# Two Gram products of the later chunk pairs moved behind an inverse product, and their copies split over ScalarE and VectorE

## The reference

```
# 1. delta-rule attention, k normalised, state S per batch and head
for t in range(S):
    y[t] = q[t] @ state
    state += beta[t] * outer(k_n[t], v[t] - k_n[t] @ state)
# 2. feed forward with three input matrices
x2 = max(x @ w1, x @ w2, x @ w3) @ w_out
# 3. mixture of 8 experts, top 2 by noisy gate
out[token] += weight * (relu(x2[token] @ we1[e]) @ we2[e])
```

## Time and profile before

| | us |
|---|---|
| median of 3 runs (1025.57 to 1025.75) | 1025.73 |
| the profiled execution's own time | 1025.56 |
| its span, first to last instruction | 1023.8 |
| attention ahead of the loop, about | 0 to 67 |
| loop over the tiles, about | 67 to 521 |
| experts | 521 to 1024 |

### The profile page before, as it was taken

One profiled execution on the slowest core, in us unless ns is written; L12 is line 12 of the kernel. 1 busy time (PEld: TensorE's weight loads), 2 busy tenths in 40 slices (PEclk: granted clock), 3 DMA queues, 4 the chain that ended last, 5 costly groups with the idle time before them and its releaser, 6 DMA issues.

```text
span 1023.8 us, 25726 instructions
## 1 busy us (share of the span) xinstructions
PE 997.9 (97%) x10425; PEld 929.1 (91%) x10425; DVE 721.6 (70%) x1701; ACT 469.7 (46%) x700; POOL 214.8 (21%) x229
## 2 busy tenths in 40 slices
PE   8899999999999999999999999999999999999995
PEld 7888898898888888888899999999999999999995
DVE  7988795893884786543569677778677686776772
ACT  4542345226325325233363546546465465654651
POOL 0464310210120130121315221212211112212111
PEclk8899999999999999999999999999999999999998
DMA  9540320420430330116656625234352526526221
GB/s 306 129 109 2 94 53 23 129 61 3 126 85 3 78 93 2 57 42 217 220 188 179 186 43 169 47 88 122 53 156 47 170 39 172 163 55 169 40 30 24
DMA packets 71190, 101.68 MB, mean 99 GB/s; under 512 B 28608, under 2 KB 59584, under 8 KB 70720
## 3 DMA queue, kind: packets, MB, share of 16 engines
q1 hardware_dynamic: 59024, 78.10, 25.4%
q0 software_dynamic: 10992, 20.70, 10.5%
q10 hardware_dynamic: 1088, 1.65, 0.5%
HBM read 136.98 MB, written 29.51 MB: 163 GB/s over the span
## 4 chain that ended last, share of the span: by engine, by line
PE 92%; DVE 3%; ACT 3%; issue 2%; POOLq 0%; POOL 0%; ACTq 0%; DVEq 0%
PE ps L1895 43%; PE ps L2061 20%; PE ps L1944 8%; PE ps L1744 3%; PE ps L2072 3%; PE ps L1874 2%; PE ps L1850 2%; PE ps L1725 2%; PE ps L1862 2%; PE ps L1960 2%; PE ps L1784 1%; DVE prod L1176 1%; DVE x L1180 1%; PE ps L1830 1%; ACT solve L862 1%
## 5 line engine op out<-in xcount | busy, mean ns | idle before, releaser
L1895 PE MATMUL ps<-xr,wr_in 128*128 128x512 f32 x972 | 235.8, 396 | 0.3 <-ACT xr L888 0.3
L1895 PEld LDWEIGHTS ps<-xr,wr_in 128*128 128x128 f32 x972 | 178.6, 188 | 39.6 <-DVE wr_in L1298 0.5
L1895 PE MATMUL ps<-xbT,w1r 128*128 128x256 f32 x1728 | 211.6, 283 | 0.6
L1895 PEld LDWEIGHTS ps<-xbT,w1r 128*128 128x128 f32 x1728 | 209.7, 192 | 2.5 <-issue 2.1
L2061 PE MATMUL ps<-w2r,hbT 128*128 128x384 f32 x1152 | 205.9, 336 | 0.0
L2061 PEld LDWEIGHTS ps<-w2r,hbT 128*128 128x128 f32 x1152 | 198.9, 188 | 0.0
L754 POOL DMA_INDIRECT out_rows<-yb,idx x55 | 91.5, 1664 | 374.8 <-DVE yb L1524 289.1
L965 ACT ACTIVATE hbT<-ps 128x512 fp32r<-128x512 f32 x96 | 57.3, 597 | 166.6 <-PE ps L1895 163.4
L1336 DVE TENSOR_TENSOR w1r<-w1s,w1r 128x768 fp32r<-128x768 f32 x124 | 117.3, 956 | 17.2 <-ACT w1r L949 15.1
L949 ACT CAST w1r<-w1s 128x768 fp32r<-128x768 f32 x124 | 101.2, 828 | 24.8 <-DMA w1s<-in_we 24.8
L1336 DVE TENSOR_TENSOR w2r<-w2s,w2r 128x768 fp32r<-128x768 f32 x124 | 110.2, 950 | 2.0 <-ACT w2r L953 2.0
(11 more groups left out here) (232 smaller groups left out, 1125.6 us busy)
## 6 DMA issues: line engine op xcount, KB each, us to landing
w1s<-in_we SPq DMA_DIRECT2D x31, 1536.0 KB
w2s<-in_we SPq DMA_DIRECT2D x31, 1536.0 KB
xb<-rows SPq DMA_DIRECT2D x24, 402.0 KB
kv_s<-in_kv SPq DMA_DIRECT2D x24, 384.0 KB, 3.7
k_s<-in_k SPq DMA_DIRECT2D x12, 512.0 KB, 4.0
joint<-in_q SPq DMA_DIRECT2D x24, 256.0 KB
out_rows<-padrow SPq DMA_DIRECT2D x13, 384.0 KB, 4.3
w_in<-in_w_blocks SPq DMA_DIRECT2D x3, 1152.0 KB, 9.7
```

What stands on the lines that cost most here:

```text
L1895: mm = pe.matmul(dst, w, m, start=(opens and n == 0), stop=(closes and n == len(todo) - 1))
```

## The change

In every pass that has them, both Gram products of the next pair stand directly behind an inverse product: behind `low_times_inverse(1)` in pass 0 (place 10), behind `corner(cp)` in passes 1 to 3 (place 2). From chunk 4 on even chunks write banks 6 and 7 (`D_BANKS`), odd ones banks 2 and 3 (`C_BANKS`), and the two waits of `gram` go. VectorE copies the blocks of the even chunk, in later passes at place 3, and ScalarE those of the odd one at the corner's place. In pass 0 who copies what, and where it stands, remains. The numbers of semaphore waits inside the copies follow, and `scaled_v` and the start of the early elimination steps are written by other names at the same places.

```diff
         def gram_banks(c):
-            return {1: H_BANKS, 2: H_BANKS, 3: D_BANKS, 4: D_BANKS, 5: C_BANKS}.get(c, E_BANKS)
+            if c < 4:
+                return (E_BANKS, H_BANKS, H_BANKS, D_BANKS)[c]
+            return C_BANKS if c % 2 else D_BANKS
...
-            spread = {"low": 1, "corner": 2, "gram0": 3, "gram1": 4, "k0": 5, "u0": 7, "s0": 8, "k1": 10, "u1": 12,
+            spread = {"low": 1, "corner": 2, "gram": 2, "k0": 5, "u0": 7, "s0": 8, "k1": 10, "u1": 12,
                       "s1": 13}
-            tight = {"low": 1, "corner": 2, "gram0": -1, "gram1": 0, "k0": 4, "u0": 5, "s0": 6, "k1": 7, "u1": 8,
+            tight = {"low": 1, "corner": 2, "gram": 1, "k0": 4, "u0": 5, "s0": 6, "k1": 7, "u1": 8,
                      "s1": 9}
...
-            low, first = place(n - 1, "low"), place(n - 2, "gram1") + 4
+            low, first = place(n - 1, "low"), place(n - 2, "corner") + 6
...
# ScalarE
-                act.wait_ge(s_blk, c + 1 if c < 4 else c)
+                act.wait_ge(s_blk, c + 1 if c < 4 else c // 2 + 3)
...
                         if i == place(t, "corner"):
                             corner(cp)
-                            if t == 0:
-                                diagonals_of(5)
-                        if t and i == place(t, "gram0") and cp + 1 < CP:
-                            diagonals_of(c + 2)
-                        if t and i == place(t, "gram1") and cp + 1 < CP:
-                            diagonals_of(c + 3)
+                            if cp + 1 < CP:
+                                diagonals_of(c + 3)
...
# VectorE
-                dve.wait_ge(s_half_diag, 3)
+                dve.wait_ge(s_half_diag, c // 2 + 1)
...
-                    if t == 0 and i == place(t, "corner"):
-                        diagonals_of(4)
+                    if i == place(t, "corner") + (1 if t else 0) and cp + 1 < CP:
+                        diagonals_of(c + 2)
...
-                        if i == place(t, "gram1"):
+                        if i == place(t, "corner") + (2 if t else -2):
                             scaled_v(c)
...
# TensorE, gram(c)
-                if c >= 6:
-                    pe.wait_ge(s_diag, c)
-                if c >= 6 and c % 2 == 0:
-                    pe.wait_ge(s_corner, c // 2 * 2)
...
-                        if i == place(t, "gram0") and cp + 1 < CP:
+                        if i == place(t, "gram") and cp + 1 < CP:
                             gram(c + 2)
-                        if i == place(t, "gram1") and cp + 1 < CP:
                             gram(c + 3)
```

## The result

The change makes the kernel slower: 1028.57 us median of 13 runs (1027.13 to 1034.01) against 1025.46 of 13 runs of the kernel before (1024.71 to 1026.27) beside it. The ratio is 1.0035, 95% interval 1.0022 to 1.0049, so about 3.1 us or 0.3 to 0.4 in a hundred. The profiled execution took 1028.57 us with a span of 1026.8, which is 3.0 more than the span before.

A forecast was written before the change was run, and what follows sets the result against it. TensorE, busy for 97% of the span, was taken to bound the kernel. Three passes winning 0.85 us each and pass 0 losing 2.95 gave +0.4 on 1025.73, so 1026.1 us; range 1023.9 to 1028.8.

The forecast's parts named there:

- pass 0's wait: Pass 0: TensorE idles 2.1 us for VectorE's inverse; corner ends at 103.7 instead of 101.3, a loss of 2.40 us.
- what passes 1 to 3 could win: Passes 1 to 3: waits go and products 3 to 5 run together, 1.40 us a pass, net 1.33.
- 0.07 for the shape: Each burst: cost of a direct change between small tile shapes, 0.07 us, bounds 0 to 0.1.
- the refill: Each of four bursts: TensorE stalls for an instruction refill due every 128 pairs or so, 0.48 us, bounds 0 to 1.1.
- The 4.2 us between refills: Refill spacing read from stalls ahead of the loop, 4.0 and 4.4 us apart; sets the refill's upper bound of 1.1 us.
- the step on the clock: Pass 0: the sum had a loss of 2.95 us and no cost for a clock fall.
- a rival with a chance of 0.14: Pass 0: idle stretch halves TensorE's clock, costing 1.6 to 1.7 us more; 1027.8 to 1028 us, chance 0.14.
- refills at their full spacing: Rival: each of four bursts stalls 1.1 us; +2.9 us in all, 1028.6 us, chance 0.14.
- The call: Whole kernel: no measurable change (under 0.2%, 2.05 us) had 0.60, slower 0.28, faster 0.12.

The follow-up runs named there:

- p0_warm7: Changed kernel plus seven matmuls of ones ahead of low_times_inverse(1) in pass 0: 1022.67 us against 1024.77 for the kernel before, ratio 0.9987.
- p0_warm14: Changed kernel plus fourteen matmuls of ones (28 in the trace) ahead of low_times_inverse(1) in pass 0: 1019.19 us against 1019.62 for the kernel before, ratio 0.9990.
- shift33: Changed kernel plus 33 tiny matmuls (66 in the trace) ahead of the loop: 1023.42 us against 1019.62 for the kernel before, ratio 1.0041.
- p0_before_shift14: Changed kernel with pass 0's Gram products back at places 8 and 9, plus 14 tiny matmuls ahead of the loop: 1021.19 us against 1024.77, ratio 0.9968.
- p0_warm3: Changed kernel plus three matmuls of ones ahead of low_times_inverse(1) in pass 0: 1020.34 us against 1019.54 for the kernel before, ratio 1.0005.
- before_shift33: Kernel before plus 33 tiny matmuls (66 in the trace) ahead of the loop: 1027.04 us against 1024.59, ratio 1.0020.
- p0_only: Kernel before with only pass 0's Gram products moved behind low_times_inverse(1): 1023.89 us against 1019.62, ratio 1.0043.
- p0_before_shift33: Changed kernel with pass 0's Gram products back at places 8 and 9, plus 33 tiny matmuls ahead of the loop: 1021.67 us against 1024.59, ratio 0.9971.

## Why the prediction was right and wrong

*Right: pass 0's wait.* Products 9 and 10 behind VectorE, a stretch of some 2 us ahead of the low product, its start at 93.1: 93.06 was measured, and with the clock kept up (p0_warm7) the corner ended at 103.56, where I had 103.7.

*Right: what passes 1 to 3 could win.* I had 1.40 us a pass less 0.07 for the shape; without stalls they win 1.53. The 0.07 was not there. Two Gram groups in one go take 3.92 us, less than twice 2.01.

*Mis-sized: the refill.* I had 0.48 us in each of four bursts. The stalls measured in passes 1 to 3 were 0.26, 0.77 and 0.72 us, mean 0.58. What they cost is more than the gap: the passes take 0.53, 1.02 and 0.94 us longer than the 10.59 without a stall, mean 0.83, inside the bounds of 0 to 1.1. In pass 0 none showed in the changed kernel: at half clock its matmuls are so late that the packet, there at 96.35 us, came 3.6 us ahead of the place where p0_warm14 stalls. The gain of the three passes was 2.1 us for 2.55. The 4.2 us between refills, on which the upper bound rests, were too many: in the changed kernel's own trace two packets began 3.47 us apart. Its cause was read rightly off, and the Trainium skill's rule that crossing a block of instructions is mostly hidden ("Runtime: NRT & Kernel Launch", Instruction fetch mechanics) does not hold for these bursts of small matmuls: single crossings stall for up to 0.95 us in the loop (shift33) and 1.66 us ahead of it (p0_before_shift14). The same section of the Trainium skill gives TensorE room for 2048 instructions, eight such blocks; by that the stream would be far ahead wherever wide products run before and between the bursts, and the stalls in the bursts of passes 1 to 3 speak against it.

*Wrong: the step on the clock.* The forecast took pass 0's loss as 2.95 us, with the clock up, and left the fall to a rival with a chance of 0.14: in the sum it stood at nothing. It fell in the profiled execution and, to judge by mean clock and time, in every one of the 13 runs. And the rival's price, 1.7 us, rested on a fall of 3.2 us as in the earlier trace rows, a stretch that I had myself cut out of the trace; the fall here lasted 6.8 us and cost 2.94. With what was measured the sum is 2.26 + 2.94 - 2.1 = +3.1, and +3.1 is what the medians show. I had placed the new idle stretch between a row where the clock fell (0.87 busy of 3.30) and one where it stayed (1.95 of 3.00) and stopped there. The row behind which it stayed up was no safe mark either: it has 1.05 us of idle time, p0_warm3 shows that with 1.10 us the clock falls in some executions, and in before_shift33 it fell behind a wait of 0.82 us. What sets the price is how long the half clock lasts and what stands there: here 6.8 us, all of small tiles that TensorE had no slack for. Whether wide products in their place would have kept it up, no run tests.

The time of 1028.57 us lies in the range, near its upper end of 1028.8, and that is luck. The end was set by refills at their full spacing, a rival whose 1028.6 is the measured time to the digit, but for another reason: in its account pass 0 stalls for a refill and the other passes win 0.23 us each, and measured were no stall in pass 0 and 0.5 to 1.0 us. The call was missed, since slower by over 0.2% had 0.28 and no change 0.60.

*A stall that didn't come.* By the count of matmuls p0_warm7 should stall 66 matmuls into the Gram group of pass 0, where p0_warm14 does 52 in. The packets tell them apart: p0_warm7's ended at 95.87 us and the matmul in question started at 97.18, 1.31 us behind, so there was nothing left to wait for; p0_warm14's came only at 97.39, and its stall ended at 98.83.

*Open.* Why two of 13 runs of the changed kernel took 1033.5 and 1034.0, with a mean clock of 0.980. And why the packet of p0_warm14 set out 1.2 us later than p0_warm7's.

## What to carry to other kernels

Before a filler is moved out of a wait, ask what TensorE's clock does in the hole: here the hole cost 2.3 us and the half clock behind it 2.9, and seven matmuls whose result nobody reads took the second away. Check each pass by itself: the same edit won 1.0 to 0.5 us where nothing was late and lost 5.2 in the one pass where VectorE's inverse was, and leaving that pass out turned +3.1 us into -2.3, measured on another chip. Where small matmuls are packed into one burst, stalls can hang on their place in the instruction stream, and a few tiny matmuls far ahead can move them under wide ones.

## What the runs showed of the hardware

- With TensorE idle for 1.75 us in front of small tiles the mean clock was lower in all 13 executions of the changed kernel and in four of five of p0_only; with 1.10 us in 6 of 10. The kernel before has it in 5 of 77. The fall lasted 6.8 us in the profile. Ahead of the loop, in before_shift33, the clock fell for 3.4 us behind a wait of 0.82 us (busy for 1.51 of the last 2.30 us), and in p0_before_shift33 it stayed at 1.00 behind one of 0.70 us (2.12 of 2.30).
- The stalls in the bursts wait for nothing that the profile's waits show, and reach 0.95 us in the loop. They move one for one with inserted matmuls (14 against 52 matmuls in, for 66 against 28 inserted), and end 1.25 to 1.60 us behind the end of a packet of the instruction queue. Its packets of 16 KB began at least 3.37 us apart in all 14 profiles.
- 14 tiny matmuls in an idle stretch ahead of the loop cost nothing that shows in the kernel before (ratio 1.0001), while 33 cost 2.4 us: they ran at half clock and past the idle time there, and the clock fell once more behind them in the profiled execution.
